# A delta-rule attention kernel: the turning of the queries moved in the schedule, A u0 multiplied in column halves, a weight split moved by one chunk

## The reference

```python
for t in range(S):                                   # attention, state (B, H, D, D)
    y[:, :, t] = einsum('bhd,bhde->bhe', q[:, :, t], state)
    v_old = einsum('bhde,bhd->bhe', state, kt)       # kt: the normalized key
    state = state + bt * einsum('bhd,bhe->bhde', kt, vt - v_old)
for e in range(E):                                   # experts
    out += p[:, e:e + 1] * (maximum(x @ w1[e], 0.0) @ w2[e])
(sigmoid(x @ w_gate) * (x @ w_val)) @ w_out          # gated layer
```

## Time and profile before

| | |
|---|---|
| median of 3 runs | 1708.73 us (1707.78, 1708.73, 1711.89) |
| the profiled execution's own time | 1704.52 us |
| its span | 1702.7 us |
| attention's slots in it | from about 24 us to about 480 us |
| experts in it | from about 523 us to about 1234 us |
| steady slot in it | 37.87 us |

### The profile page before, as it was taken

How to read it: one execution, slowest core, us unless ns; L and a number is a source line. 1 busy time by engine, 2 the same in 40 slices (tenths; PEclk the granted TensorE clock), 3 DMA queues, 4 the chain that set the end, 5 groups by cost and what they waited for, 6 DMA issues and landing times. The chain is left out here.

```text
span 1702.7 us, 35068 instructions
## 1 busy us (share of the span) xinstructions
PE 1632.3 (96%) x14630; PEld 1462.4 (86%) x14630; DVE 654.5 (38%) x1193; ACT 436.1 (26%) x852; POOL 279.3 (16%) x404
## 2 busy tenths in 40 slices
PE   5899999999988999999999999999989999999999
PEld 4788888888877899999999999999878888888887
DVE  5777777777632232222222222222243222222221
ACT  3333334444312212211121111111143222222222
POOL 4654444444300300300003000000000000000000
PEclk9999999999999999999999999999999999999999
DMA  6335433344137241111212112211030000000000
GB/s 136 66 89 136 98 96 91 89 99 98 49 110 279 86 156 66 38 64 48 111 37 75 37 37 67 73 38 37 0 112 29 19 19 1 19 0 18 0 19 19
DMA packets 171731, 113.23 MB, mean 66 GB/s; under 512 B 82224, under 2 KB 151216, under 8 KB 171600
## 3 DMA queue, kind: packets, MB, share of 16 engines
q1 hardware_dynamic: 171600, 111.33, 22.2%
HBM read 92.43 MB, written 18.87 MB: 65 GB/s over the span
## 5 line engine op out<-in xcount | busy, mean ns | idle before, releaser
L1165 DVE SCALAR_TENSOR_TENSOR hl<-ebank,hh 128x512 fp32r<-128x512 f32 x168 | 116.4, 693 | 503.8 <-ACT hh L1130 503.8
L1130 ACT ACTIVATE hh<-ebank 128x512 fp32r<-128x512 f32 x168 | 100.6, 599 | 577.9 <-PE ebank L1196 577.9
L1194 PE MATMUL ebank<-w2l,hh 128*128 128x384 f32 x672 | 226.4, 337 | 3.8 <-DVE hl L1165 3.8
L1196 PE MATMUL ebank<-w2h,hh 128*128 128x384 f32 x672 | 226.6, 337 | 0.0
L1195 PE MATMUL ebank<-w2h,hl 128*128 128x384 f32 x672 | 225.9, 336 | 0.0
L1194 PEld LDWEIGHTS ebank<-w2l,hh 128*128 128x128 f32 x672 | 126.4, 188 | 10.7 <-DVE hl L1165 4.2
L1195 PEld LDWEIGHTS ebank<-w2h,hl 128*128 128x128 f32 x672 | 126.3, 188 | 6.0
L1390 DVE TENSOR_TENSOR prod<-gbank,gate 128x512 f32<-128x512 f32 x72 | 49.7, 690 | 209.6 <-ACT gate L1337 209.6
L1196 PEld LDWEIGHTS ebank<-w2h,hh 128*128 128x128 f32 x672 | 126.3, 188 | 0.0
L1315 POOL COPY stage<-acc 128x1536 f32 (+1 forms) x5 | 7.4, 1475 | 601.5 <-POOLq L1056 323.6
L1194 PE MATMUL ebank<-room,w1h 128*128 128x512 f32 x252 | 99.3, 394 | 4.3 <-DVE w1l L1152 4.3
(11 more groups left out here) (175 smaller groups left out, 3313.4 us busy)
## 6 DMA issues: line engine op xcount, KB each, us to landing
room<-x_hi SPq DMA_DIRECT2D x12, 768.0 KB, 4.2
room<-x_lo SPq DMA_DIRECT2D x12, 768.0 KB, 5.7
xh<-x_hi SPq DMA_DIRECT2D x12, 768.0 KB, 4.2
xl<-x_lo SPq DMA_DIRECT2D x12, 768.0 KB, 5.8
brep<-in_beta SPq DMA_DIRECT2D x24, 256.0 KB, 5.7
k_raw<-in_k SPq DMA_DIRECT2D x12, 384.0 KB, 4.0
v_raw<-in_v SPq DMA_DIRECT2D x12, 384.0 KB, 5.7
q<-in_q SPq DMA_DIRECT2D x12, 384.0 KB, 6.2
```

Source lines behind the costliest of these rows:

```text
L1130: nc.scalar.activation(hs[i][0][:, :], bank[i][:, :], ACT.Relu).then_inc(hh_done, 1)
L1165: nc.vector.scalar_tensor_tensor(out=hs[i][1][:, :], in0=bank[i][:, :], scalar=0.0, in1=hs[i][0][:, :].bitcast(F32), op0=ALU.max, op1=ALU. ...
L1194: mm(dst, stat[0], mov[1], start=first, stop=False)
L1196: return mm(dst, stat[0], mov[0], start=False, stop=last)
```

## The change

`turn_q` of window w is taken from the end of slot w − 1 and put into slot w, its first half behind `au_a` 0 and its second behind `au_b` 0 of window w − 1's recurrence. `down` 2 and 3 go from behind the second `product_q` to ahead of it. A head's A is multiplied in two halves of 64 columns, each into its own 64 partitions. ScalarE splits the weights of expert 1 in the third chunk of expert 0 and no longer in the second; the other experts keep theirs.

```diff
--- before.py
+++ after.py
@@ -240,10 +240,12 @@
             n("unit", 0)
             n("unit", 1)
             r("au_a", 0)
+            pre("turn_q", w, p, 0)
             up(0)
             moe("low", m, 0)
             both("l3")
             r("au_b", 0)
+            pre("turn_q", w, p, 1)
             up(1)
             moe("low", m, 1)
             both("l4")
@@ -272,18 +274,16 @@
             r("y", 1)
             pre("product_q", w, p, 0)
             r("s", 0)
+            down(m, 0, 2, 3)
             pre("product_q", w, p, 1)
-            down(m, 0, 2, 3)
             r("s", 1)
             n("first", 0)
             n("first", 1)
-            n("turn_q", 0)
-            n("turn_q", 1)
 
         def run(lev, rec, pre, moe):
             for step, which in (("square", None), ("norm", None), ("unit", 0), ("unit", 1),
                                 ("turn", 0), ("turn", 1), ("product", 0), ("product", 1),
-                                ("first", 0), ("first", 1), ("turn_q", 0), ("turn_q", 1)):
+                                ("first", 0), ("first", 1)):
                 pre(step, 0, 0, which)
             for w in range(NW):
                 slot(w, w % 2, lev, rec, pre, moe)
@@ -822,6 +822,13 @@
                                       start=True, stop=True)
                         last.then_inc(mz_rdy, 1)
 
+                def halves(out, o, heads, stat, mov):
+
+                    for h in heads:
+                        for qs in (slice(0, DP), slice(DP, P)):
+                            last = mm(thin(out)[qs, h, :], stat[:, HH * o + h, qs], mov[:, h, :], start=True, stop=True)
+                    return last
+
                 def rec(step, w, p, o):
                     out = rbank[o]
                     if step == "z":
@@ -850,13 +857,9 @@
                         last.then_inc(u0_rdy, 1)
                     if step == "au_a":
                         pe.wait_ge(u0_done, 2 * w + o + 1)
-                        for h in range(HH // 2):
-                            mm(thin(out)[:, h, :], A32[p][:, HH * o + h, :], U0[o][:, h, :], start=True, stop=True)
+                        halves(out, o, range(HH // 2), A32[p], U0[o])
                     if step == "au_b":
-                        for h in range(HH // 2, HH):
-                            last = mm(thin(out)[:, h, :], A32[p][:, HH * o + h, :], U0[o][:, h, :],
-                                      start=True, stop=True)
-                        last.then_inc(au_rdy, 1)
+                        halves(out, o, range(HH // 2, HH), A32[p], U0[o]).then_inc(au_rdy, 1)
                     if step == "u2":
                         pe.wait_ge(r2_done, 2 * w + o + 1)
                         if w < NW - 1:
@@ -1139,9 +1142,11 @@
                 for f in range(KH):
                     split1(0, f)
                 for e in range(E):
-                    chunk(NCK * e, e)
-                    chunk(NCK * e + 1, e, e + 1 if e + 1 < E else None)
-                    with act.Fori(NCK * e + 2, NCK * (e + 1)) as g:
+                    turn = 2 if e == 0 else 1
+                    for c in range(turn):
+                        chunk(NCK * e + c, e)
+                    chunk(NCK * e + turn, e, e + 1 if e + 1 < E else None)
+                    with act.Fori(NCK * e + turn + 1, NCK * (e + 1)) as g:
                         chunk(g, e)
 
             @block.vector
```

## The result

| | before | after |
|---|---|---|
| median of 20 runs each | 1708.61 us (1696.31 to 1722.12) | 1715.67 us (1711.83 to 1724.35) |
| profiled execution | 1704.52 us | 1712.70 us |
| its span | 1702.7 us | 1710.9 us |
| mean granted clock of it | 0.987 | 0.969 |

The ratio is 1.0055, with a 95% interval of 1.0031 to 1.0080. The change makes the kernel 0.55% slower where I had forecast 0.7% faster, and 1715.67 us lies outside my range of 1686 to 1708.

A forecast was written before the change was run, and what follows sets the result against it. TensorE's work plus its waits was taken as the bound (busy 96%). Terms −8.8 − 1.2 − 5.7 + 4.4 = −11.3 us took the profiled execution from 1704.5 to 1693.2, the median from 1708.7 to 1697 us; range 1686 to 1708.

The forecast's parts named there:

- the clock's: New 2.1 us gap ahead of l0: three short falls to a lower TensorE clock, 1.5 us each, +4.4 us.
- the harmless case: Stretch after 474.80, 1.99 of 3.50 us busy among products, where the granted clock stays at 1.00.
- the long fall in every slot: Gap ahead of l0 leaves TensorE at 1.2 GHz each slot: 11 x 2.95 us, 1726 us in all; chance 0.06.
- The end of a slot: From `s` 0 to l0: `down` covers the masks, 0.3 us gained, TensorE idle 2.1 us in one piece.
- The queries in their new place: Between l2 and l4: 0.46 us of TensorE per half, about 0.2 us of it filling l4's wait.
- ScalarE's late copies: Second query copy delays the last level's copies by up to 0.6 us; costed at nothing, otherwise 6.6 us in all.
- A u0 in halves: A four-head group hands on after 0.61 us instead of 0.91, gaining 0.30 us; four groups a slot.
- the row of `s`: Profile row of an `s` group, same shape and count as halved A u0, handing on after 0.61 us.
- The rival without overlap: A u0 halves do not overlap, so groups gain nothing: 13.2 us less gain, 1710 us; chance 0.07.
- A quiet slot: Steady slot of 37.87 us without the clock's term: −0.8 us a slot, −8.8 us over 11 slots.
- The later split: Expert 0's second chunk loses ScalarE's 4.79 us wait for w2 and the low clock after it: −5.7 us.
- The last slot: No `s` 0 covers `product_q` 1 there; six products of `down` fill its wait: −1.2 us.

The follow-up runs named there:

- down_split: The changed kernel with `down` 2 between the two `product_q` and `down` 3 behind `s` 1, gap ahead of l0 1.26 us; 1707.40 us, ratio 1.0013.
- gap_mid: The kernel before with column halves, the later split and both `product_q` ahead of `s` 0, so TensorE idles between products; 1693.88 us, ratio 0.9929.
- turn_only: The changed kernel without column halves and later split, leaving the moved query turning and slot-end order; 1732.86 us, ratio 1.0165 to the kernel before.
- halves_only: The kernel before with A u0 in column halves and nothing else; 1693.02 us, ratio 0.9949.
- fill16: The changed kernel with 16 unread products of 256 float16 columns in TensorE's gap ahead of l0; 1680.61 us, ratio 0.9871 to the kernel before.

## Why the prediction was wrong

**The step that failed is the clock's.** I had written: "I take three short ones, +4.4 us, since the gap's other neighbour is `s` and `product_q`, like the harmless case." The runs show that idle time just ahead of l0 is not like the harmless case (down_split against gap_mid). Ten slots of ten fell, seven of them long. A long fall lasts about 10 us and costs some 4.0 us a slot (41.0 against 37.0), more than the 2.95 that I had for one: my row was a slot whose fall lasts about 7 us, and I took its extra busy time instead of its extra length of 3.5. Without the clock's term my sum was −15.7 us. The measured +7 makes that term about +23 us on top of the falls that the kernel before has of its own, against the +4.4 that I took.

**The rival that happened** is the first one, the long fall in every slot, to which I gave 0.06. I had put its point of decision at the sixth slot with 2.95 us each; at 4.0 us each it is the fourth. Its mechanism came true, its 1726 us did not: three of the falls were short, and the kernel before already pays for falls of its own. I had the evidence on the page: the fall after 447.50 began at a stall beside the small tiles, and the stretch without a fall had its stall among the products. I read it rightly as a difference of place and then put the new gap, which touches both, on the harmless side without a row that spoke for it. No row before the change shows a gap of that size with dense work ahead of it and small tiles behind.

**The end of a slot** was right. The gap is 1.98 us for 2.1, the end is 0.4 us shorter for the 0.3 that I had, and it is VectorE's masks and additions that are late.

**The queries in their new place** cost 0.41 us a half where I had 0.46. In a quiet slot of turn_only all the moved steps together are worth +0.1 us, where my terms gave about +0.4. ScalarE's late copies, which I had costed at nothing, show no cost in it.

**A u0 in halves** was right for the group. A group hands on after 0.60 us in the changed kernel (348.66 to 349.26 in its timeline) for the 0.61 of the row of `s`. The rival without overlap is refuted. What reaches the slot depends on VectorE: 0.5 us in halves_only, where it is late at l4. The Trainium skill's page "TensorEngine Tiling (Array Packing)", section "Key Properties", lets one expect a drain at each change of mode; if there is one here it lies within the 0.60 us.

**A quiet slot** takes 36.97 us (in fill16) for 37.87, so −0.9 where I had −0.8.

**The later split** was right within the stage: −5.7 us in the profiled execution. As a difference of medians it could not be shown.

**The last slot**: the longest wait of a `product_q` for the masks went from 1.53 us there to at most 0.8. Its worth of 1.2 us was not tested by itself.

## What to carry to other kernels

A change that gathers idle time into one gap on TensorE is to be judged by what stands behind the gap, not by the sum of the waits. Put dense work, real if there is some, between a long wait and a stretch of small tiles. And when the clock is what moves the time, compare slots of one profiled execution at a clock of 1.00 with each other first, since that gives the worth of the schedule apart from the clock.

## What the runs showed of the hardware that was not expected

- Sixteen products that nobody reads, 1.92 us a slot of pure addition in a gap, made the changed kernel 1.8% faster (ratios of 1.0055 and 0.9871 to the same kernel before; 1715.67 and 1680.61 us in different series).
- A gap of 1.26 us ahead of l0's 32x32 tiles took the clock down in nine slots of nine, in eight of them for about 10 us; one of 1.53 us between products in 64x128 tiles did it in one slot of nine, for 3.5 us.
- After a gap of 2 us the granted clock stayed down for about 10.4 us in seven slots of ten and for about 3.5 in three. In the slot shown that is the stretch that holds l0, l1 and l2, though TensorE was busy for 10.29 of 10.37 us there. How far the sparse tiles themselves keep it down was not tried.
